# VectorE's order in the first pair of each channel stage, with late low parts on GpSimd and the last outer products in block order

## The reference

```python
def _moe2_ref(x, g_ln, w_ch1, w_ch2) -> np.ndarray:
    mu = np.mean(x, axis=-1, keepdims=True)
    var = np.mean((x - mu) ** 2, axis=-1, keepdims=True)
    xn = (x - mu) / np.sqrt(var + 1e-06) * g_ln
    ch = np.maximum(xn @ w_ch1, 0.0) @ w_ch2
    return (x + ch).astype(np.float32)
```

## Time and profile before

| | us |
|---|---|
| median of 3 runs | 690.5 (690.43 to 690.56) |
| the profiled execution, its own time | 689.21 |
| its span, first to last instruction | 686.7 |
| TensorE busy | 658.4 |
| VectorE busy | 484.8 |
| ScalarE busy | 347.7 |
| GpSimd busy | 344.9 |

### The profile page before, as it was taken

One profiled execution on the slowest core, in us unless ns is written; L12 is line 12 of the kernel. 1 busy time (PEld: TensorE's weight loads), 2 busy tenths in 40 slices (PEclk: granted clock), 3 DMA queues, 4 the chain that ended last, 5 costly groups with the idle time before them and its releaser, 6 DMA issues.

```text
span 686.7 us, 12380 instructions
## 1 busy us (share of the span) xinstructions
PE 658.4 (96%) x3719; PEld 580.1 (84%) x3719; DVE 484.8 (71%) x1003; ACT 347.7 (51%) x775; POOL 344.9 (50%) x319
## 2 busy tenths in 40 slices
PE   6899999999999999999999997999999989999997
PEld 3788788888888897999889986899889778898896
DVE  5999999999999974534645588655555896556534
ACT  3788888888888983411344342522233523232210
POOL 4987778887555514000001044665568765666530
PEclk9999999999999999999999999999999999999999
DMA  7543434454333002000000011121111123112002
GB/s 250 182 124 116 135 120 142 144 154 124 92 92 93 24 2 85 0 1 1 1 0 1 1 62 61 48 76 63 61 61 62 62 94 122 62 66 94 25 0 93
DMA packets 18709, 51.41 MB, mean 75 GB/s; under 512 B 2481, under 2 KB 4657, under 8 KB 18673
## 3 DMA queue, kind: packets, MB, share of 16 engines
q1 hardware_dynamic: 17328, 45.45, 20.1%
q0 software_dynamic: 1344, 5.51, 2.6%
HBM read 47.75 MB, written 3.19 MB: 74 GB/s over the span
## 4 chain that ended last, share of the span: by engine, by line
PE 65%; DVE 15%; issue 15%; DVEq 1%; ACT 1%; ACTq 0%
PE bank L578 19%; PE bank L580 18%; PE bank L579 18%; DVE PTl L1224 6%; DVE negated L1204 3%; PE bank L628 3%; PE bank L640 1%; PE bank L642 1%; DVE Q L1177 1%; PE bank L597 1%; PE bank L596 1%; PE bank L651 1%; DVE BL L1334 1%; PE bank L695 1%; DVE den L1230 0%
## 5 line engine op out<-in xcount | busy, mean ns | idle before, releaser
L956 ACT ACTIVATE Pe<-bank,neg_max 128x768 f32<-128x768 f32 x96 | 87.1, 907 | 29.6 <-DVE negated L1204 29.2
L1204 DVE TENSOR_SCALAR_CACHE_REDUCE negated<-bank 128x768 bf16<-128x768 f32 x96 | 91.5, 954 | 12.9 <-PE bank L597 9.5
L1224 DVE TENSOR_TENSOR PTl<-bank,PTh 128x384 fp32r<-128x384 f32 x192 | 97.5, 548 | 2.3 <-ACT PTh L951 1.8
L628 PE MATMUL bank<-cst,Pe 128*128 128x128 f32 x576 | 85.6, 280 | 8.8 <-DVE PTl L1224 8.6
L951 ACT ACTIVATE PTh<-bank 128x384 fp32r<-128x384 f32 x192 | 86.3, 494 | 7.6 <-PE bank L628 7.5
L628 PEld LDWEIGHTS bank<-cst,Pe 128*128 128x128 f32 x576 | 64.3, 140 | 26.3 <-DVE PTl L1224 14.0
L578 PE MATMUL bank<-BH,W1H 128*128 128x384 f32 x224 | 76.1, 340 | 7.9 <-DVE U4s L1365 3.8
L578 PE MATMUL bank<-W2H,Hh 128*128 128x512 f32 x192 | 75.9, 395 | 2.3 <-issue 1.2
L579 PE MATMUL bank<-W2L,Hh 128*128 128x512 f32 x192 | 75.9, 395 | 0.0
L580 PE MATMUL bank<-W2H,Hl 128*128 128x512 f32 x192 | 75.6, 394 | 0.0
L580 PE MATMUL bank<-BH,W1L 128*128 128x384 f32 x224 | 75.4, 336 | 0.0
(11 more groups left out here) (152 smaller groups left out, 1572.0 us busy)
## 6 DMA issues: line engine op xcount, KB each, us to landing
w_pair<-w_ch SPq DMA_DIRECT2D x16, 1024.0 KB, 4.9
q_raw<-qqT SPq DMA_DIRECT2D x16, 384.0 KB, 5.1
k_raw<-kkT SPq DMA_DIRECT2D x16, 384.0 KB, 5.6
qk_raw<-qkT SPq DMA_DIRECT2D x15, 384.0 KB, 3.2
v_raw<-v SPq DMA_DIRECT2D x16, 192.0 KB, 4.6
out<-X SPq DMA_DIRECT2D x12, 256.0 KB, 2.1
rows<-code_rows SPq DMA_DIRECT2D x15, 192.0 KB, 4.6
w_raw<-w_spT POOLq DMA_DIRECT2D x6, 384.0 KB, 3.5
```

The source lines that it names most:

```text
L628: last = nc.tensor.transpose(bank[:, PT_BANK + j, r * P:(r + 1) * P], Pe[n % 2][:, k * P:(k + 1) * P], ident)
L956: nc.scalar.activation(Pe[n % 2][:, :].rearrange("p (c n) -> p c n", c=2), bank[:, 2 * (n % 2):2 * (n % 2) + 2, 0:C], ACT.Exp, bias=neg_ma ...
L1204: nc.vector.tensor_scalar(halves(negated[:, :]), bank[:, 2 * (n % 2):2 * (n % 2) + 2, 0:C], -SCALE, 3.0e38, ALU.mult, ALU.min, accum_out=n ...
L1224: nc.vector.tensor_tensor(PTl[m][part], bank[:, PT_BANK + j, 0:C].rearrange("p (k q) -> p k q", k=HC), f32(PTh[m][part]), ALU.subtract).th ...
```

## The change

Five things are altered.

1. VectorE's order in a pair. In pair 0 (`xns`) the normalisations of the last three `XN` tiles, `Hl` and the four sums for `W1` stood together between `U2s` and `U4s`; now each addition stands as early as it can, the three normalisations between them, and all `Hl` and the sums behind `C12s`. In pair 7 (`operands`) the `BL` are spread, one behind each of four additions. In pair 8 (`adds`) the final additions stand later.
2. ScalarE's order follows: in pair 0 the units of `XNT` are copied one by one, from product 0 on, and all four `W1H` of pair 1 are rounded at the end of the pair.
3. GpSimd makes T1 to T4 of a batch one behind the other: T3 in place in `XNT`, T4 in a buffer of its own, `T4s` (for batch 0 once the spatial product is done). It also makes the low parts 4 to 6 of batch 1, behind its work for pair 7.
4. TensorE does the last outer products of a batch in block order, like all others.
5. The two last `BL` of batch 0 stand between the statistics of `Y`.

```diff
-        T_SUM = {2: 1, 3: 0, 4: 2, 5: 3}
-        T_BLOCK = {0: (0, 0), 1: (1, 0), 6: (1, 1)}
+        EARLY = 4
+        T_COUNT = {2: 2, 3: 1, 4: 3, 5: 4}
...
+        def operand(i):
+
+            return (block_of(0, 0), block_of(1, 0), Tsum[1][:, :, :], Tsum[0][:, :, :], block_of(0, 1), T4s[:, :, :],
+                    block_of(1, 1))[i]
...
-            def t_sums_12(b):
+            def t_sums(b):
...
                 nc.gpsimd.tensor_tensor(Tsum[1][:, :, :], block_of(1, 1), Tsum[0][:, :, :], ALU.subtract).then_inc(t_sum, 1)
-
-            def t_sums_34(b):
-
-                pool.wait_ge(b_lo, PRODUCTS * b + 4)
-                nc.gpsimd.tensor_tensor(Tsum[0][:, :, :], block_of(1, 1), block_of(0, 1), ALU.subtract).then_inc(t_sum, 1)
-                nc.gpsimd.tensor_tensor(Tsum[1][:, :, :], block_of(1, 0), Tsum[1][:, :, :], ALU.subtract).then_inc(t_sum, 1)
+                pool.wait_ge(t_sum, 4 * b + 2)
+                nc.gpsimd.tensor_tensor(block_of(0, 1), block_of(1, 1), block_of(0, 1), ALU.subtract).then_inc(t_sum, 1)
+                if b == 0:
+                    pool.wait_ge(s_mm, 2 * KU * B)
+                nc.gpsimd.tensor_tensor(T4s[:, :, :], block_of(1, 0), Tsum[1][:, :, :], ALU.subtract).then_inc(t_sum, 1)
...
                 if b == 0:
-                    t_sums_34(1)
+                    for i in range(EARLY, PRODUCTS):
+                        pool.wait_ge(b_hi, PRODUCTS + i + 1)
+                        lo_of(BL[i][:, :, :], operand(i), BH[i][:, :, :], b_late_lo)
...
                     if beside == "xn":
-                        last_xn_units(((), (), (), (), range(4), range(4, 6), range(6, 8))[i])
-                    elif beside == "final":
-                        if i < T:
-                            final_tile(g, 1 - s, i)
+                        last_xn_units(((0,), (1,), (2,), (3,), (4, 5), (6,), (7,))[i])
                     else:
                         out_groups(b, g, 1 - s, range((0, 2, 4, 6, 8, 10, 11)[i], (2, 4, 6, 8, 10, 11, 12)[i]),
-                                   beside == "first")
+                                   beside == "first", beside == "final")
...
-            for t in range(T):
-                final_tile(NPR * B, 1, t)
+            out_groups(B, NPR * B, 1, range(4 * HC), final=True)
...
                 copy_p1(g, s)
-                prepare(0)
+                turned(0)
                 if operands:
                     operand_hi(b + 1, 0)
+                if not xns:
+                    prepare(0)
...
                 if operands:
-                    for i in range(4, PRODUCTS):
-                        operand_hi(b + 1, i)
+                    operand_hi(b + 1, 6)
+                turned(7)
                 if xns:
-                    for u in range(6, 8):
-                        xn(1, u, LAST_XN_BANKS[u])
-                    prepare(2)
-                    prepare(3)
+                    for i in range(4):
+                        prepare(i)
```

More of the change, by code:

```diff
@@ L808, in product, with out_groups @@
                 last.then_inc(p_mm, 1)
-            def out_groups(b, g, s, which, first):
+            def out_groups(b, g, s, which, first=False, final=False):
                 for q in which:
@@ L825, in out_groups @@
                     last = three(bank[:, t, :], Hh[s][:, f, tok], Hl[s][:, f, tok], W2H[s][:, f, :], W2L[s][:, f, :],
-                                 first and n < 2, False)
+                                 first and n < 2, final and n >= 2)
                     if q == 4 * HC - 1:
                         last.then_inc(w2_done, 1)
[L830 to L840, removed]
+                    elif final and n >= 2:
+                        last.then_inc(out_mm, 1)
             def last_xn_units(which):
@@ L1051, in prepare, with turned @@
                         w1_high(g + 1, 1 - s, i, loads)
+                def turned(*which):
+                    if xns:
+                        for u in which:
+                            xn(1, u, LAST_XN_BANKS[u])
                 copy_p1(g, s)
-                prepare(0)
+                turned(0)
                 if operands:
                     operand_hi(b + 1, 0)
+                if not xns:
+                    prepare(0)
                 act.wait_ge(added, START + 7 * g + 1)
@@ L1071, in channel_pair @@
                 hidden_hi(s, 1, 1, C22s)
-                if xns:
-                    for u in range(4):
-                        xn(1, u, LAST_XN_BANKS[u])
+                if operands:
+                    operand_hi(b + 1, 4)
+                turned(4, 5)
                 act.wait_ge(added, START + 7 * g + 6)
@@ L1077, in channel_pair @@
                 hidden_hi(s, 1, 0, C21s)
-                if xns:
-                    for u in range(4, 6):
-                        xn(1, u, LAST_XN_BANKS[u])
+                if operands:
+                    operand_hi(b + 1, 5)
+                turned(6)
                 act.wait_ge(added, START + 7 * g + 7)
@@ L1390, in channel_pair @@
                 add(U2s, s, 2, P1s)
-                hidden_low(g, s, 0, 0, 0, C11s)
                 if xns:
                     y_inverse_root(b + 1, 1)
-                    y_normalise(b + 1, 1)
-                    w1_sum_1(g + 1, 1 - s, loads)
-                    w1_sum_2(g + 1, 1 - s)
-                if more:
-                    w1_sum_3(g + 1, 1 - s)
-                    w1_sum_4(g + 1, 1 - s)
-                if operands:
-                    for i in range(3):
-                        operand_low(b + 1, i)
-                if adds:
-                    final_add(b - 1, 1)
-                    final_add(b - 1, 2)
+                else:
+                    hidden_low(g, s, 0, 0, 0, C11s)
+                    if more:
+                        w1_sum_3(g + 1, 1 - s)
+                        w1_sum_4(g + 1, 1 - s)
+                low_operand(1)
                 dve.wait_ge(p_mm, 7 * g + 4)
@@ L1420, in channel_pair @@
                 add(U3s, s, 4, U2s)
[L1421 removed]
+                if xns:
+                    y_normalise(b + 1, HC + 1)
+                    y_normalise(b + 1, HC + 2)
+                else:
+                    hidden_low(g, s, 1, 1, 1, C22s)
+                low_operand(3)
                 if adds:
[L1423 removed]
+                    final_add(b - 1, 0)
+                    final_add(b - 1, 1)
                 dve.wait_ge(p_mm, 7 * g + 6)
@@ L1433, in channel_pair @@
                 add(C12s, s, 6, U4s)
+                if xns:
+                    hidden_low(g, s, 0, 0, 0, C11s)
+                    hidden_low(g, s, 1, 1, 1, C22s)
                 hidden_low(g, s, 2, 1, 0, C21s)
+                if adds:
+                    final_add(b - 1, 4)
                 hidden_low(g, s, 3, 0, 1, C12s)
-                if operands:
-                    for i in range(4, PRODUCTS):
-                        operand_low(b + 1, i)
+                if xns:
+                    w1_sum_1(g + 1, 1 - s, loads)
+                    w1_sum_2(g + 1, 1 - s)
+                    w1_sum_3(g + 1, 1 - s)
+                    w1_sum_4(g + 1, 1 - s)
+                if adds:
+                    final_add(b - 1, 5)
             def final_add(b, t):
@@ L1493, in mlp @@
                     w1_sum_4(0, 0)
-                    for i in range(5, PRODUCTS):
-                        operand_low(0, i)
                 for t in range(HC):
                     y_stats(b, t)
+                    if b == B - 1 and t < 2:
+                        operand_low(0, 5 + t)
                 variance(slice(0, HC), T * b + HC, y_mv, y_var)
                 y_inverse_root(b, 0)
-                y_normalise(b, 0)
+                for t in range(HC):
+                    y_normalise(b, t)
                 for t in range(HC, T):
@@ L1507, in mlp @@
                     y_inverse_root(b, 1)
-                    y_normalise(b, 1)
+                    for t in range(HC, T):
+                        y_normalise(b, t)
             def channel(b):
```

81 lines of the change are left out of this document (39 added, 42 removed).

## The result

The changed kernel took 702.3 us (median of 4 runs, 700.9 to 703.5), the kernel before 690.5 beside it: a ratio of 1.0173, 95% interval 1.0153 to 1.0194. The forecast was 691.6 with a range up to 693.3, so it was wrong. The profiled execution took 701.5 us with a span of 699.4 and a mean granted clock of 0.985; before it was 686.7, and the clock was full.

The account below looks back on a forecast made before the run. TensorE, busy 96% of the span, was taken as the bound, so only its waits count, with VectorE and GpSimd taking turns on SBUF; +1.5 + 1.0 - 0.9 - 0.6 = +1.0 us gave 691.5 to 691.6, range 686.9 to 693.3.

Parts of the forecast that it names:

- Third Tsum, early: MLP step: GpSimd's T3 of batch 0 right behind T2 makes VectorE's normalisation and TensorE 1.5 us later; bounds 0 and 1.9.
- Pair 0, products 2 to 6: Pair 0: TensorE waits from 425.4 to 427.8 before units 4 and 5; product 5 starts at 428.45 against 429.24.
- The first W1H goes to the end of pair 0: Pair 0's end: W1L comes late, product 0 of pair 1 starts about 435.1, not 432.70; pair 0 in all costs 1.0 us.
- The 2.14 before product 2: Pair 0: the last two BL between the statistics bring product 2 0.35 us earlier; bounds 0 and 1.2.
- Pairs 7 and 8: VectorE and GpSimd taking turns: stalls of 4.7 us become 3.8, a gain of 0.9; bounds 4.1 and -1.
- The end: Last outer products in block order: the 0.62 us wait goes, 0.6 us gained after store costs; bounds 0.1 and 0.8.
- In pair 8 I find none: Pair 8: no stalls; C11s ends at 554.5, product 3 is due at 555.3, U4s ends 0.5 before product 5.
- I count idle time plus 0.3 for each stall: TensorE's waits: pricing rule, each stall costs its idle time plus 0.3 us.
- The rivals: Whole kernel: order wins, 686.8 us (chance 0.20); half of it, 689.5 (0.15); slower, 693.3 (0.08).
- the third: Rival, pair 8: GpSimd's three BL make C11s 1.9 us late, +1.8 on the sum, 693.3 us; chance 0.08.

Follow-up runs that it names:

- t34_late: Changed kernel, but GpSimd makes the third and fourth sums of batch 1 behind its low parts in pair 7, not ahead: 701.9 us, ratio 1.0167.
- lows_later: three_undone, with VectorE's BL 1, 2 and 3 each one step later in pair 7: 687.2 us, ratio 0.9954.
- load_first: Changed kernel, but SyncE issues the load of pair 10's weights ahead of the six stores of batch 0: 696.1 us, ratio 1.0075.
- pair8_back: Changed kernel, with pair 8's outer products and final additions put back to their old places: 696.3 us, ratio 1.0089.
- t3_late: Changed kernel, but GpSimd waits for all low parts of V of batch 1 before T3 of batch 0: 699.0 us, ratio 1.0124.
- all_four: three_undone together with t34_late: 688.6 us, ratio 0.9978.
- w1h_early: Changed kernel, but ScalarE rounds the first two W1H of pair 1 early in pair 0, as before: 696.2 us, ratio 1.0069.
- three_undone: Changed kernel with load_first, t3_late and w1h_early together, the rest of the change kept: 688.1 us, ratio 0.9971.
- lows_xn: lows_later, with the second of pair 0's last three XN ahead of C22s and U3s: 687.5 us, ratio 0.9955.

## Why the prediction was wrong

The prediction's sum was +1.0 for the median, and the measurement says +11.8. By its own steps:

- *Third Tsum, early.* Right, in place, cause and size: +1.5 was forecast, +1.53 measured, and the wait of about 2 us stands where it was said to. VectorE got its turn one operation later than I wrote (at rstd, not at the last rs).
- *Pair 0, products 2 to 6*, and *The first W1H goes to the end of pair 0*. Right: 2.25 us before units 4 and 5 (2.4 forecast), 3.80 before product 0 of pair 1 (3.5 to 4), and +1.0 to +1.1 in all once the half clock is taken off (+1.0 forecast). *The 2.14 before product 2* became 1.24, and product 2 comes 0.25 earlier against product 0 (0.35 forecast).
- *Pairs 7 and 8.* The net gain was right (0.71 measured, 0.9 forecast), the way to it only in part: before product 5 TensorE waits 1.51, not 2.6, before product 6 0.39, not 0.7, and the 0.91 for C21s of pair 8 was not forecast at all. These errors cancel, so the right net figure is partly luck. The sum of 3.8 also counts the 0.3 of a restart once for three stalls; by its own rule it would be some 4.3, and the gain 0.4. t34_late shows that GpSimd's order leaves the sum of these waits as it is, and lows_later that VectorE's own order sets what TensorE sees of it.
- *The end.* Right, 0.75 for 0.6.
- **The step that failed** is where *Pairs 7 and 8* ends, at "In pair 8 I find none". The final additions, which the change moves later in pair 8, have no term in the sum, and neither have the stores and the load behind them; pair 9 isn't looked at. Their cost was put at nothing without a reason, and it was 3.9 us of wait and 2.5 of clock. I followed what waits for VectorE on TensorE, and not what waits for it on SyncE: the stores wait for the additions, and the load of pair 10 stands behind the stores. The row was there before, as VectorE's 2.54 us for w_pair at 570.80, right ahead of a C11s with 0.16 us to spare. Taking the load out of that queue gave back 6.2 us (load_first), and making the additions early gave back 6.0 (pair8_back).
- **The second failure** is the price of a stall. "I count idle time plus 0.3 for each stall" left out the clock. The waits of 2.02, 3.80 and 3.89 cost about 1.5, 1.6 and 2.5 us more at half clock. I had taken it from one wait of the kernel before, the 2.00 in pair 8, behind which the clock stayed full, as it did behind the 2.14 and 2.75 there. That undoing a wait also undoes the fall of the clock is shown by t3_late and load_first.
- The remaining 1.9 of the profiled difference is nearly all there by 60 us (1.8), in a stretch which the change leaves alone: the granted clock is 0.83 from 10 to 20 us and 0.96 from 20 to 60, where the kernel before had 1.00. It comes and goes between executions (last section).

The two failures account for the miss: 3.9 of wait in pair 9 and 5.6 of clock are 9.5. The steps that were forecast sum to 1.5 + 1.1 - 0.7 - 0.75 = 1.15, and 1.9 stands ahead of them all. Together that is 12.6 of the 12.7 of span. This adds up one execution; in another the clock's share can differ by some us (last section). The rivals didn't have it either: the third put its loss into pair 8, by another mechanism.

As to what the change was worth: the later final additions gained nothing in pair 8 (0.57 us of waits gone, 0.91 new) and cost 6.2 through SyncE. The gain in pairs 7 and 8 is left for moving the late BL off VectorE, which no run tried alone. With the three harmful moves undone the rest is 0.3% faster than the kernel before, and with the low parts one step later 0.5%.

## What to carry to other kernels

When an operation is moved later, list everything that waits for it on every queue, the DMA queue too, and then what stands behind that in the same queue: a load behind a store is as late as the store's data. Allow, as a bound, a stretch at half clock around each new stall of about 2 us or more (here it cost 1.5 to 2.6 us, and nothing around some), and look for it in windows of the granted clock, since a list of waits doesn't show it. Where two engines take turns at the memory, changing GpSimd's order here only moved the wait (t34_late); what helped was to take the contended operations out of the chain that TensorE waits for (lows_later).

## What the runs showed of the hardware

- TensorE's clock fell to 1.2 GHz around waits of 2.02, 3.80 and 3.89 us, and stayed full around 2.14 and 2.75 in the kernel before and around 2.20 in t34_late and all_four. The same wait of 2.25 us before the last transposes was followed by a full clock in the changed kernel, t3_late and t34_late, and by a lower one in load_first, pair8_back, w1h_early, three_undone, all_four and lows_later; in lows_xn one followed a wait of 1.90. Its length alone doesn't decide.
- So the price of the same stalls differs between traces. From product 2 of pair 0 to C11s of pair 2, with the same waits of 2.25 and 3.80 us (3.75 in pair8_back), the stretch is 2.9 us longer than in the kernel before in the changed kernel and in t34_late, 3.9 in t3_late, 5.5 in load_first and 5.6 in pair8_back.
- An operation of VectorE on six numbers per partition took 1.69 us beside one of GpSimd and 0.17 without it.
- The start differs between executions by as much as the largest edits gain: GpSimd's first Tsum, which no step of the change touches, starts between 359.0 and 364.7 us in the twelve traces. Where it is late, the clock is lower in the first 60 us: 0.75 from 10 to 20 us in all_four (364.7), 0.83 in w1h_early (362.1), 1.00 in the kernel before (359.0). Differences below 1 us were read here between two instructions inside one trace, and compared with the same two in another.
